# A mixed recurrence and expert kernel: the opening in another order, gating by two wide products, loads and early weight splits re-planned

## The chip, the cores and the metric

The kernel runs on one core of a Trainium2 chip. The metric is the device time in microseconds (us), taken as the median of several executions.

## What is computed

Two stages. The first is a gated recurrence (B = 2, H = 8, S = 768, D = 40), the second a dense mixture of four experts (1536 tokens, 320 to 1024 to 320 columns):

```python
m_new = max(f[t] + m, i[t]); f_stab = exp(f[t] + m - m_new); i_stab = exp(i[t] - m_new)
C = f_stab * C + i_stab * outer(v[t], k[t]);  n = f_stab * n + i_stab * k[t]
y[t] = sigmoid(o_gate[t]) * (C @ q[t]) / max(abs(n @ q[t]), 1.0)

x = y, heads side by side: (1536, 320);  p = domain_probs / (sum(domain_probs) + 1e-9)
out = sum over e of p[:, e] * (relu(x @ w1[e]) @ w2[e])
```

## The kernel before

**Units.** The tokens are cut into NT = 12 units of L = 128 (a chunk of one batch, all eight heads). Units 0 and 1 are the first chunks of the two batches and have no earlier state. For a unit k, `decays` (ScalarE) computes exponentials of gate sums into dec_w, one half being four heads; `causal` (GpSimd) masks them; `scores` (TensorE) multiplies queries and keys; `probs` (VectorE, DVE) multiplies scores and decays; `outputs` (TensorE) multiplies by the values, and from unit 2 on adds the part of the carried state; `additions` makes what the unit adds to the state from kw, which `weigh_keys` (GpSimd) prepares. `denominator` and `gate_x` (DVE) divide, and multiply by the sigmoid of the output gate, which `gate_open` (ScalarE) writes in place in y_acc. `transpose_x` turns the result; `xt_high` (ScalarE) and `xt_low` (DVE) split it into a high and a low part for products in reduced-precision fp32.

**Experts.** The weights of one expert are eight blocks of 128 hidden columns; a pair of blocks (704 KB) is one transfer into w_raw, which holds RAW_PAIRS = 3 pairs. `split_high` (ScalarE) rounds a block to w_hi, `split_low` (GpSimd) takes the rest in two pieces, 384 columns for the up product and 320 for the down product. Work is cut into SLOTS = 128 slots, sixteen groups of eight; the first three groups have two units each. In a slot M, `up(M+2)` (later M+1) makes the hidden values (eight matmuls, for two units of 256 columns), `relu` (ScalarE) and `hidden_low` (DVE) split them, and `down(M)` adds to acc_ps. After the eighth slot of a group `add_expert` (DVE) puts acc_ps into y_acc.

**Order.** Each engine runs a list written by hand, in order; semaphores tie the lists together. T0 says at which slot a unit starts (unit 2 at 3, unit 3 at 7, unit 4 at 16): its decays run at slots T0-1 and T0, the scores at T0 and T0+2, additions and outputs at T0+3, gate_x at T0+4, transposes at T0+6. EARLY_SPLITS says which weight blocks are split in slots 0 to 5. All loads but one are issued by SyncE (SP), so a wait in its list holds up every load behind it. Weight pair p waits until w_lo_done says that the pair three before it is split.

**The opening.** SyncE issues the gates, the scores' operands of units 0 and 1, keys and values, o_gate of units 0 to 3 (one transfer), and weight pair 0. `gate_steps` and `gate_sums` make the gate sums, first for units 0 and 1 (16 rows, gate tiles 0) and then for the ten others (80 rows, gate tiles 1), whose running maximum comes by five small transfers into m_u. TensorE runs `keep_clock` products, matmuls whose result is not used, between the steps. ScalarE holds one table of functions at a time; going from Exp to Sigmoid or back is an ACT_TABLE_LOAD. The second o_gate transfer (units 4 to 11, 1280 KB) lands on y_acc[:, 4:NT], where the gates of the opening lie until m_moved.

## Time and profile before

| | |
|---|---|
| median of 3 runs | 444.98 us (443.33 to 447.54) |
| the profiled execution | 445.01 us, span 443.3 us |
| TensorE (PE) busy | 97% of the span |
| VectorE (DVE), ScalarE (ACT), GpSimd (POOL) busy | 40%, 37%, 37% |
| read from and written to HBM | 44.79 MB, 2.05 MB |

Times in the trace count from the start of the span. PE is the matmul, PEld the weight load beside it; SPq is SyncE's queue. A number such as L908 is a line of the kernel: L908 is the up product, L925 down, L866 and L874 outputs, L847 additions, L820 scores, L886 to L888 the transposes, L789 keep_clock, L464 a decay, L613 probs, L644 gate_x, L384 and L386 the two pieces of split_low, L623 the split of queries and keys, L694 add_expert, L308 the second o_gate transfer. The granted clock is given as a share of the full clock.

### The profile page before, as it was taken

The page shows a single profiled execution, that of the slowest core. Times are in us where ns is not written, and L with a number is a line of the kernel's source. Part 1 is how long each engine was busy: PE and PEld are TensorE (multiplying, and loading weights), DVE is VectorE, ACT ScalarE, POOL GpSimd, SP SyncE. Part 2 cuts the span into 40 slices and gives each one's busy share as a digit, 9 for nine tenths or more (in the row PEclk, how much of TensorE's full clock was granted, in tenths as well). Part 3 has the DMA queues.
Part 4 walks back from the last instruction along what each step waited for, and adds up shares of the span by engine and source line. Part 5 has one row for each costly group of instructions (what it writes and reads, how often), then busy time and mean ns, then how long its engine had stood idle before and what let it go on. Part 6 is the DMA issues. An engine that isn't in the chain of part 4 may idle for free.

```text
span 443.3 us, 7101 instructions
## 1 busy us (share of the span) xinstructions
PE 429.0 (97%) x2716; PEld 412.8 (93%) x2716; DVE 175.9 (40%) x419; ACT 164.1 (37%) x332; POOL 164.3 (37%) x193
## 2 busy tenths in 40 slices
PE   8998689999999999999999999999999999999997
PEld 7887689999999999999999999999999999999996
DVE  6632144656564465653724323232313223122132
ACT  3656337557344382542412243124311233111111
POOL 4538763469453585521301066006500145100000
PEclk9899779999999999999999999999999999999999
DMA  8769688826985159740000024102220010001010
GB/s 234 236 182 267 248 241 241 203 65 172 288 187 151 67 149 257 189 138 6 0 1 1 0 74 136 53 0 92 106 67 0 1 65 1 0 1 59 1 59 31
DMA packets 25589, 47.33 MB, mean 107 GB/s; under 512 B 1971, under 2 KB 18788, under 8 KB 24468
## 3 DMA queue, kind: packets, MB, share of 16 engines
q1 hardware_dynamic: 25412, 46.86, 37.1%
q8 instruction: 22, 0.36, 0.3%
q14 instruction: 11, 0.09, 0.1%
q10 hardware_dynamic: 144, 0.02, 0.0%
HBM read 44.79 MB, written 2.05 MB: 106 GB/s over the span
## 4 chain that ended last, share of the span: by engine, by line
PE 87%; DMA 4%; DVE 3%; SPq 3%; ACT 1%; issue 1%; POOL 1%; DVEq 0%; ACTq 0%
PE hid_ps L908 38%; PE acc_ps L925 32%; PE out_ps L866 4%; PE score_ps L925 3%; PE add_ps L847 2%; DMA w_raw<-in_w_b 2%; PE out_ps L874 2%; PE score_ps L825 1%; PE hid_ps L789 1%; DMA raw<-in_qk_a 1%; PE score_ps L820 1%; DMA m_u<-y_acc 1%; SPq L308 1%; PE acc_ps L908 1%; DVE prob L613 1%
## 5 line engine op out<-in xcount | busy, mean ns | idle before, releaser
L678 DVE SCALAR_TENSOR_TENSOR h_lo<-hid_ps,h_hi 128x384 fp32r<-128x384 f32 (+2 forms) x120 | 68.0, 566 | 243.2 <-ACT h_hi L499 243.1
L499 ACT ACTIVATE h_hi<-hid_ps 128x384 fp32r<-128x384 f32 (+2 forms) x120 | 59.8, 498 | 246.5 <-PE hid_ps L908 246.0
L925 PE MATMUL acc_ps<-w_hi,h_hi 128*128 128x320 f32 x352 | 110.9, 315 | 1.3 <-DVE y_acc L694 1.2
L925 PE MATMUL acc_ps<-w_hi,h_lo 128*128 128x320 f32 x352 | 108.8, 309 | 0.0
L925 PE MATMUL acc_ps<-w_lo,h_hi 128*128 128x320 f32 x352 | 108.5, 308 | 0.0
L908 PE MATMUL hid_ps<-xt_hi,w_hi 128*128 128x384 f32 (+2 forms) x360 | 104.8, 345 | 2.4 <-issue 1.7
L384 POOL TENSOR_TENSOR w_lo<-w_raw,w_hi 128x384 fp32r<-128x384 f32 x56 | 61.1, 1091 | 117.6 <-ACT w_hi L485 117.6
L908 PE MATMUL hid_ps<-xt_hi,w_lo 128*128 128x384 f32 (+2 forms) x360 | 102.3, 341 | 0.0
L908 PEld LDWEIGHTS hid_ps<-xt_hi,w_lo 128*128 128x128 f32 x360 | 65.7, 190 | 4.0
L925 PEld LDWEIGHTS acc_ps<-w_hi,h_hi 128*128 128x128 f32 x352 | 66.5, 189 | 3.1 <-issue 1.4
L925 PEld LDWEIGHTS acc_ps<-w_lo,h_hi 128*128 128x128 f32 x352 | 66.4, 189 | 1.4
L908 PEld LDWEIGHTS hid_ps<-xt_hi,w_hi 128*128 128x128 f32 x360 | 62.6, 189 | 4.7 <-issue 2.4
L925 PEld LDWEIGHTS acc_ps<-w_hi,h_lo 128*128 128x128 f32 x352 | 66.2, 188 | 0.0
L908 PE MATMUL hid_ps<-xt_lo,w_hi 128*128 128x384 f32 (+2 forms) x240 | 63.0, 343 | 0.0
L386 POOL TENSOR_TENSOR w_lo<-w_raw,w_hi 128x320 fp32r<-128x320 f32 x56 | 50.0, 893 | 0.0
L485 ACT ACTIVATE w_hi<-w_raw 128x704 fp32r<-128x704 f32 x56 | 43.6, 782 | 6.4 <-DMA w_raw<-in_w_b 6.4
L908 PEld LDWEIGHTS hid_ps<-xt_lo,w_hi 128*128 128x128 f32 x240 | 43.0, 190 | 2.9
L364 POOL TENSOR_SCALAR_AFFINE_SELECT dec_w<-dec_w 128x512 f32<-128x512 f32 x24 | 15.3, 636 | 68.2 <-ACT dec_w L464 68.2
L866 PEld LDWEIGHTS out_ps<-kv,prob 128*128 128x128 f32 x176 | 22.7, 206 | 3.7 <-DVE prob L613 3.7
L866 PE MATMUL out_ps<-kv,prob 128*128 128x41 f32 x176 | 22.7, 306 | 3.4 <-DVE prob L613 3.4
L464 ACT ACTIVATE dec_w<-g_all,w_tok 128x128 f32<-128x128 f32 x80 | 25.4, 391 | 0.0
L623 DVE TENSOR_TENSOR split_qk<-raw,split_qk 40x1024 fp32r<-40x1024 f32 x16 | 22.4, 1398 | 0.2
(156 smaller groups left out, 384.2 us busy)
## 6 DMA issues: line engine op xcount, KB each, us to landing
w_raw<-in_w_b SPq DMA_DIRECT2D x28, 704.0 KB, 4.7
raw<-in_qk_s SPq DMA_DIRECT2D x8, 960.0 KB
g_all<-g_dram SPq DMA_DIRECT2D x10, 512.0 KB, 9.1
kv<-in_kv_n SPq DMA_DIRECT2D x12, 320.0 KB, 7.1
out_y<-y_acc SPq DMA_DIRECT2D x12, 160.0 KB, 1.9
q_pack<-in_q_p SPq DMA_DIRECT2D x10, 180.0 KB, 9.3
carry<-g_dram SPq DMA_DIRECT2D x30, 60.0 KB
y_acc<-in_o_n SPq DMA_DIRECT2D x1, 1280.0 KB, 12.0
```

Source lines behind the costliest of these rows:

```text
L364: nc.gpsimd.affine_select(out=d, in_=d, compare_op=ALU.is_ge, fill=0.0, base=0, pattern=[[0, HALF], [1, L]], channel_multiplier=-1).then_i ...
L384: nc.gpsimd.tensor_tensor(w_lo[:, f, 0:384], w_raw[:, at, 0:384], w_hi[:, f, 0:384].bitcast(fp32), ALU.subtract)
L386: nc.gpsimd.tensor_tensor(w_lo[:, f, 384:WB], w_raw[:, at, 384:WB], w_hi[:, f, 384:WB].bitcast(fp32), ALU.subtract).then_inc(w_lo_done, 1)
L464: last = nc.scalar.activation(dec_w[:, half, a, :], e, ACT.Exp, bias=w_tok[:, k * H + h:k * H + h + 1])
L485: nc.scalar.activation(w_hi[:, f, :], w_raw[:, at, :], ACT.Copy).then_inc(w_hi_done, 1)
L499: nc.scalar.activation(h_hi[:, M % RING, 0:cols], hid_bank(M)[:, 0:cols], ACT.Relu).then_inc(hid_hi, 1)
L623: nc.vector.tensor_tensor(hi, raw[rows, kept(k), t, :, :], hi.bitcast(fp32), ALU.subtract)\
L678: nc.vector.scalar_tensor_tensor(h_lo[:, M % RING, 0:cols], hid_bank(M)[:, 0:cols], 0.0, h_hi[:, M % RING, 0:cols].bitcast(fp32), ALU.max, ...
L847: last = nc.tensor.matmul(bank[0:KS, first * DA:(first + n) * DA], kw[:, kept(k), KS * g:KS * (g + 1)], values(k, first, n), start=True, s ...
L866: last = nc.tensor.matmul(bank[:, h * DA:(h + 1) * DA], prob[:, kept(k), h // HALF, h % HALF, :], values(k, h, 1).rearrange("p h e -> p (h ...
L908: last = nc.tensor.matmul(hid_bank(M)[:, 0:tiles * L], w, x, start=(i == 0), stop=(i == len(terms) - 1))
L925: last = nc.tensor.matmul(acc_ps[t][:, 0:DM], x, w, start=(f == 0 and i == 0), stop=(f == NF - 1 and i == 2))
```

## The change

- SyncE: o_gate of units 0 to 3 comes in two transfers right behind the gates. Weight pair 2 moves ahead of the scores' operands of unit 2; those of unit 3 and q of unit 3 move up behind them, and keys and values of unit 2, with their waits for out_done and add_done, ahead of pair 3. Keys and values of unit 3 stand ahead of g 2, and g 3 behind pair 4. The second o_gate transfer moves to slot 9, pairs 8, 9 and 10 to slots 12, 14 and 16, and a unit's loads from its slot T0+5 to T0+6.
- ScalarE: the sigmoids of units 0 to 3 come first, then the exponentials. Unit 1's decays go into g_all[:, 1], so they no longer wait for unit 0's products. Blocks 0 to 3 are split ahead of xt_high(0). The later sigmoids move from slots 9 and 10 to 13 and 14.
- DVE: all four products of the opening come ahead of gate_steps(1), the scan of gate_sums is a function of its own, and domain probabilities come last. `denominator` and `gate_x` are one function: one wide product with the sigmoid, one wide product with the reciprocals, instead of eight. For blocks 2 to 15 the down piece of the low part is made here (`split_down_low`), no longer on GpSimd.
- GpSimd: split_low(0) ahead of weigh_keys; blocks 2 to 15 only the up piece.
- TensorE: exponents first, scores(0,0) behind them; ten keep_clock products at the start and three later, where there were nine and twenty-two; key turn ahead of outputs(0); additions(0) and (1) behind the transposes, ahead of up(0). In `up` the low weights come ahead of the low part of x, and each is waited for where it is first used.

```diff
+DN_FIRST, DN_END = 2, 16
+LATER_PAIRS = {12: 8, 14: 9, 16: 10}
...
+        def dec(k, half):
+
+            return g_all[:, 1, half * HALF:(half + 1) * HALF, :] if k == 1 else dec_w[:, half, :, :]
...
             sp.dma_start(fi_sb, fi_rows).then_inc(gates_in, 16)
+            sp.dma_start(y_acc[:, 0:2, :], o_n[:, 0:2, :]).then_inc(o_in[0], 16)
+            sp.dma_start(y_acc[:, 2:4, :], o_n[:, 2:4, :]).then_inc(o_in[1], 16)
             load_scores(sp, 0)
             load_scores(sp, 1)
             load_kv(sp, 0)
-            sp.dma_start(y_acc[:, 0:4, :], o_n[:, 0:4, :]).then_inc(o_in[0], 16)
             load_kv(sp, 1)
 
             def load_pair(p):
 
                 wait_if(sp, w_lo_done, 2 * (p - RAW_PAIRS) + 2)
+                if halved_low(2 * (p - RAW_PAIRS)):
+                    sp.wait_ge(w_dn_done, 2 * (p - RAW_PAIRS) + 2 - DN_FIRST)
...
             load_pair(1)
+            load_pair(2)
             reload_scores(2)
             load_q(2)
-            load_pair(2)
+            reload_scores(3)
+            load_q(3)
+            sp.wait_ge(out_done, 1)
+            sp.wait_ge(add_done, 1)
+            load_kv(sp, 2)
             load_pair(3)
...
-            sp.wait_ge(out_done, 1)
-            sp.wait_ge(add_done, 1)
-            load_kv(sp, 2)
+            sp.wait_ge(out_done, 2)
+            sp.wait_ge(add_done, 2)
+            load_kv(sp, 3)
             sp.wait_ge(gate_tiles[1]["stored"], 2 * 16)
             load_g(2)
             load_carry(2)
             load_pair(4)
-            reload_scores(3)
-            sp.wait_ge(out_done, 2)
-            sp.wait_ge(add_done, 2)
-            load_kv(sp, 3)
             load_g(3)
-            load_q(3)
             load_carry(3)
-            sp.wait_ge(m_moved, 16 * (NC - 1))
-            sp.dma_start(y_acc[:, 4:NT, :], o_n[:, 4:NT, :]).then_inc(o_in[1], 16)
...
+                if M == T0[3] + 2:
+                    sp.wait_ge(m_moved, 16 * (NC - 1))
+                    sp.dma_start(y_acc[:, 4:NT, :], o_n[:, 4:NT, :]).then_inc(o_in[2], 16)
...
             causal(1, 1)
+            split_low(0)
             weigh_keys(0)
             weigh_keys(1)
-            for w in range(FIRST):
+            for w in range(1, FIRST):
                 split_low(w)
...
+            gate_open(0, 2)
+            gate_open(2, 2)
+            nc.scalar.activation(table_turn[:, 1:2], m_sb[:, 0:1], ACT.Exp)
             decays(0, 0)
...
             key_exp(0)
-            gate_open(0, 2)
             split_high(0, None)
             split_high(1, None)
+            split_high(2, None)
+            split_high(3, None)
             xt_high(0)
-            gate_open(2, 2)
             xt_high(1)
             relu(0)
-            split_high(2, None)
             relu(1)
-            split_high(3, None)
...
-            def denominator(k):
+            def gate_x(k):
+
 
                 dve.wait_ge(out_done, k + 1)
+                dve.wait_ge(sig_ready, k // 2 + 1 if k < 4 else k // 4 + 2)
+                wait_if(dve, xt_ps, k - 1)
                 total = out_bank.get(k, out_ps)[:, 0:H * DA].rearrange("p (h e) -> p h e", h=H)
+                x = x_nat[:, kept(k), :].rearrange("p (h d) -> p h d", h=H)
                 nc.vector.tensor_scalar(floor[:, :], total[:, :, D], 1.0, None, ALU.max).then_inc(floor_ready, 1)
+                nc.vector.tensor_tensor(x, total[:, :, 0:D], y_acc[:, k, :].rearrange("p (h d) -> p h d", h=H),
+                                        ALU.mult).then_inc(x_gated, 1)
...
+                nc.vector.tensor_tensor(x, x, rden[:, :].unsqueeze(2).broadcast_to([L, H, D]), ALU.mult)\
+                    .then_inc(x_ready, 1)
+
+            def split_down_low(w):
+
+                at, f = (w // 2) % RAW_PAIRS * 2 + w % 2, w % NF
+                dve.wait_ge(w_hi_done, w + 1)
+                nc.vector.tensor_tensor(w_lo[:, f, 384:WB], w_raw[:, at, 384:WB], w_hi[:, f, 384:WB].bitcast(fp32),
+                                        ALU.subtract).then_inc(w_dn_done, 1)
...
+            probs(0, 0)
+            probs(0, 1)
+            probs(1, 0)
+            probs(1, 1)
+            copy_keys(0, 0, U0, acc_ps[2])
+            dve.wait_ge(units_in, 16)
+            dve.wait_ge(m_moved, 16 * (NC - 1))
+            gate_steps(1, fi_u[:, 0, :], fi_u[:, 1, :], m_u[:, 0:L], m_u[:, 1:L + 1])
+            gate_x(0)
+            gate_scan(1)
+            gate_x(1)
+            xt_low(0)
+            xt_low(1)
+            gate_sums(1)
...
+                for w in blocks_to_split(M - 1) if M > 0 else []:
+                    if halved_low(w):
+                        split_down_low(w)
...
                 if first_of_load(M):
                     pe.wait_ge(w_hi_done, NF * load + f + 1)
-                    pe.wait_ge(w_lo_done, NF * load + f + 1)
                 if f == 0:
-                    pe.wait_ge(xt_done, first + tiles)
+                    pe.wait_ge(xt_hi_done, first + tiles)
...
                 for i, (w, x) in enumerate(terms):
+                    if i == 2 and first_of_load(M):
+                        pe.wait_ge(w_lo_done, NF * load + f + 1)
+                    if i == 4 and f == 0:
+                        pe.wait_ge(xt_done, first + tiles)
...
-            keep_clock(9)
-            scores(0, 0)
+            keep_clock(10)
             pe.wait_ge(ident_ready, 2)
             pe.wait_ge(g0["ready"], 1)
             turn(g0, "w", acc_ps[2], 0, U0, "w_ps")
             exponents_first(0, 0)
             exponents_first(0, 1)
-            scores(0, 1)
+            scores(0, 0)
             exponents_first(1, 0)
             exponents_first(1, 1)
+            scores(0, 1)
             scores(1, 0)
             scores(1, 1)
-            keep_clock(4)
-            outputs(0)
             pe.wait_ge(g0["exp"], 1)
             pe.wait_ge(g0["w_tok"], 1)
             turn(g0, "key", acc_ps[2], U0, U0, "key_ps")
-            keep_clock(4)
+            outputs(0)
             outputs(1)
             transpose_x(0)
-            keep_clock(8)
+            additions(0)
+            keep_clock(1)
             transpose_x(1)
-            keep_clock(6)
+            additions(1)
+            keep_clock(2)
             up(0)
...
             up(1)
-            additions(0)
-            additions(1)
```

## Rows read from the trace of the kernel before

**Rows 1.** The page: busy us (share of the span) xinstructions of each engine.
```profile
PE 429.0 (97%) x2716; PEld 412.8 (93%) x2716; DVE 175.9 (40%) x419; ACT 164.1 (37%) x332; POOL 164.3 (37%) x193
```

**Rows 2.** Stretches: us; busy PE, PEld, DVE, ACT, POOL (xinstructions); granted clock; DMA share; GB/s.
```profile
28.83:48.27 19.44, 17.27 (x117) 15.88 (x116) 4.27 (x12) 10.30 (x23) 14.41 (x17) 1.00 1.05 293
48.27:51.71 3.44, 0.00 (x2) 0.00 (x1) 1.08 (x3) 2.17 (x5) 1.31 (x2) 0.81 0.84 341
51.71:60.25 8.54, 8.54 (x36) 8.18 (x36) 0.75 (x3) 3.42 (x11) 5.65 (x8) 0.50 0.53 149
...
61.17:101.00 39.83, 37.04 (x281) 36.14 (x280) 22.92 (x64) 23.29 (x45) 21.30 (x24) 1.00 0.65 173
101.00:443.30 342.30, 339.37 (x2121) 327.46 (x2120) 127.95 (x275) 111.25 (x219) 107.28 (x117) 1.00 0.27 76
```

**Rows 3.** The chain that ended last, in order of time: start, us, piece; slots 8 to 14.
```profile
65.56 0.87 PE score_ps L820 x4
...
69.46 1.19 PE add_ps L847 x6
70.65 1.73 PE out_ps L866 x16
72.38 0.69 PE out_ps L874 x6
...
80.84 0.88 PE acc_ps L925 x6
81.73 0.96 PE acc_ps L908 x8
```

**Rows 4.** The timeline of the opening: start us, us, instructions; first a piece of the chain.
```profile
1.85 4.21 DMA raw<-in_qk_a
...
8.03 2.18 ACT L464 ACTIVATE dec_w<-acc_ps,w_tok 128x128 f32<-128x128 f32 x8 [5.29 <-PE acc_ps L797]
...
13.33 1.28 ACT L442 ACT_TABLE_LOAD   x1
...
15.44 1.28 DVE L613 TENSOR_TENSOR prob<-acc_ps,dec_w 128x512 f32<-128x512 f32 x2
...
16.94 1.97 PE L866 MATMUL acc_ps<-kv,prob 128*128 128x41 f32 x16 [1.09 <-DVE key_w L597]
...
17.34 1.43 DVE L644 SCALAR_TENSOR_TENSOR x_nat<-out_ps,rden,y_acc 128x40 f32<-128x40 f32 x8
...
22.18 0.42 PE L886 MATMUL acc_ps<-ident,x_nat 128*128 128x128 f32 x1
```

**Rows 5.** Busy time by single us around the first fall of the clock, columns as in rows 2.
```profile
19.00:20.00 1.00, 1.00 (x9) 1.00 (x9) 0.90 (x6) 0.59 (x2) 1.00 (x2) 0.84 0.92 323
...
23.00:24.00 1.00, 1.00 (x11) 1.00 (x10) 0.42 (x2) 0.49 (x1) 0.00 (x0) 0.95 0.87 220
```

**Rows 6.** The chain around weight pair 5, and transfers: KB each, median us to landing.
```profile
35.81 3.03 SPq L308
...
38.88 10.64 DMA w_raw<-in_w_b
...
g_all<-g_dram SPq DMA_DIRECT2D x10, 512.0 KB, 9.1
...
y_acc<-in_o_n SPq DMA_DIRECT2D x1, 1280.0 KB, 12.0
...
y_acc<-in_o_n SPq DMA_DIRECT2D x1, 640.0 KB, 6.6
```

**Rows 7.** One line's instructions (ns min/median/max), and the timeline of a collision.
```profile
L386 POOL TENSOR_TENSOR w_lo<-w_raw,w_hi x56: 850/872/1848, 19.3 to 377.5; 128x320 fp32r<-128x320 f32 x56
...
109.86 1.82 DVE L623 TENSOR_TENSOR split_qk<-raw,split_qk 40x1024 fp32r<-40x1024 f32 x1
...
110.54 2.00 POOL L384 TENSOR_TENSOR w_lo<-w_raw,w_hi 128x384 fp32r<-128x384 f32 x1
```

**Rows 8.** TensorE's waits, 24 to 110 us: who for whom, total us, times, longest.
```profile
PE acc_ps L925 <- DVE y_acc L694: 1.2, 1, 1.2
```

More of the change, by code:

```diff
@@ L181, in build @@
         gates_in, units_in, dp_in = sem("gates_in"), sem("units_in"), sem("dp_in")
-        o_in = [sem(f"o_in{i}") for i in range(2)]
+        o_in = [sem(f"o_in{i}") for i in range(3)]
         w_in = [sem(f"w_in{i}") for i in range(RAW_PAIRS)]
@@ L362, in causal @@
                 pool.sem_inc(mask_turn, 1)
-                d = dec_w[:, half, :, :]
+                d = dec(k, half)
                 nc.gpsimd.affine_select(out=d, in_=d, compare_op=ALU.is_ge, fill=0.0, base=0,
@@ L463, in decays @@
                     e = bank[:, a * L:(a + 1) * L] if k < B else g_all[:, kept(k), h, :]
-                    last = nc.scalar.activation(dec_w[:, half, a, :], e, ACT.Exp, bias=w_tok[:, k * H + h:k * H + h + 1])
+                    last = nc.scalar.activation(dec(k, half)[:, a, :], e, ACT.Exp, bias=w_tok[:, k * H + h:k * H + h + 1])
                 last.then_inc(d_exp, 1)
@@ L574, in gate_sums @@
                     .then_inc(step, 1)
+            def gate_sums(n):
+                gt = gate_tiles[n]
+                g, j, gg, step = gt["g"], gt["j"], gt["gg"], gt["step"]
                 dve.wait_ge(step, 5)
@@ L602, in _ @@
             gate_steps(0, fi_sb[:, 0, 0:L], fi_sb[:, 1, 0:L], m_sb[:, 0:L], m_sb[:, 1:L + 1])
+            gate_scan(0)
             gate_sums(0)
@@ L699, in add_expert @@
                                                        ALU.mult, ALU.add).then_inc(acc_free, 1)
+            probs(0, 0)
[12 more added lines that the diff above has]
+            gate_sums(1)
+            hidden_low(0)
+            copy_tokens(1, U0, U1, out_ps)
+            hidden_low(1)
+            keep_heads(0)
+            keep_heads(1)
+            for w in range(DN_FIRST, FIRST):
+                split_down_low(w)
             dve.wait_ge(dp_in, 16)
```

78 lines of the change are left out of this document (32 added, 46 removed).

## The prediction

> **What bounds the kernel now.** I read the busy times first: TensorE is busy for 429.0 of 443.3 us [rows 1], so only time in which it stands still or runs slowly can be won. The busy time by stretches shows where that is. From 101 us to the end it is busy for 339.37 of 342.30 us, all at full clock, and nothing in the diff shortens a matmul there. From 28.83 to 48.27 it is busy for 17.27 of 19.44; from 48.27 to 51.71 it does nothing; from 51.71 to 60.25 it is busy, but at a granted clock of 0.50, which is the lower of its two levels (1.2 GHz) [rows 2]. I call pass M of the main loop slot M. Slot 0 begins with up(2) at 28.83, slot 8 with up(10) at 61.17.
>
> What do slots 0 to 7 cost without a loss? The chain of work gives 0.96 for up, 0.88 for down, 0.87 for half the scores, and 1.19 + 1.73 + 0.69 = 3.6 for a unit's additions and outputs [rows 3]. Eight ups and downs are 14.7, three halves of scores 2.6, one unit's additions and outputs 3.6, the key turn and the diagonal product of slot 1 about 0.4 (an estimate, two or three small matmuls of the 0.23 to 0.5 kind [rows 3, 4]): 21.3 us. They took 61.17 - 28.83 = 32.3. So **11.0 us are lost**: 2.2 in small gaps before 48.27, 3.4 in the gap, 4.3 as half of the 8.54 slow us, and some 1.1 in gaps and half-clock edges around them. The last part is the difference, not read.
>
> Who causes the gap? The chain names it. SyncE was busy for 3.03 us issuing the second o_gate transfer (1280 KB) at 35.81, issued weight pair 5 behind it at 38.88, and that landed 10.64 us later, at 49.5 [rows 6]. ScalarE takes that pair in slot 4; the relus and the decays of unit 2 stand behind it in its queue, then the DVE product, then outputs(2) on TensorE. The idle time let the clock fall.
>
> **The opening, step by step.** Before: the decays run from 8.03 (eight in 2.18, so 1.1 a half), wait once for a product to free dec_w, and end with key_exp at 13.3, where the table of the sigmoid is loaded (1.28) [rows 4]. After: the two small o_gate transfers go right behind the gates, 320 KB each. The 640 KB of before took 6.6 us behind 1.2 MB of other loads; fi, 96 KB and first in the queue, and the scores' operands (416 KB) bound the other side, the latter with 4.21 us from issue to landing [rows 4, 6]. I take landings at 5.5 and 6.5. A decay of 128 columns takes 0.27, so a sigmoid of 640 takes at most five times that, 1.4, and with one fixed part instead of five about half, 0.7 (an estimate). The sigmoids end at 7.2, the exp table at 8.5, the small activation at 8.7. Decays: 8.7 to 13.1, with no wait between, since unit 1 now writes g_all. key_exp ends at 13.5. So this part is level with before: the removed wait pays for the early sigmoid. With 6.6 us per landing it would start 2.3 later.
>
> The Trainium skill, ScalarE: Activation LUTs, section Table sets: the hidden batching unit, puts a switch at about 2.7 us. This trace disagrees, with 1.28 [rows 4]; by the page the decays would begin 1.4 later and the sum below would be 1.4 higher.
>
> From there, TensorE: key turn at 13.6, outputs(0) 13.8 to 15.7 and outputs(1) right behind, to 17.6, each like the 1.97 of before; before, outputs(1) started at 16.94, because the DVE stood in front of unit 1's products waiting for m_u and did gate_steps(1) first; its two products ran at 15.44 to 16.72 [rows 4]. That is 1.3 earlier. gate_x: eight products of 1.43 together become two wide ones. A 128x512 product is half of 1.28, 0.64 to 0.69, so 320 columns are 0.45 to 0.5 each; one lies in the shadow of the floor and denominator chain, so x is ready 0.6 earlier per unit [rows 4]. x(0) is ready at 17.1, inside outputs(1), turned by 18.1. x(1): done at 17.6, gate_scan(1) in front, ready at 19.1; additions(0) fill TensorE until 19.4; turned by 20.0, where before its turn began at 22.18 after eight keep_clock products. additions(1) to 21.2, two keep_clock products, up(0) and up(1) from 21.7 to 23.7, the turn of w: slot 0 at 24.0, 4.8 before the 28.83 of now [rows 3, 4]. That includes the 2.4 us of additions that now stand after up(1).
>
> **The clock.** It fell to 0.84 in 19 to 20 and was back at 0.95 in 23 to 24, after outputs(1) and an idle us ahead of them, and in spite of the keep_clock products [rows 4, 5]. After the change there are 13 such products instead of 31, and ten of them stand at the start; from 13.6 to 21 TensorE has only narrow outputs, transposes and additions. I expect the fall. A slow stretch of 3.2 us as in 20 to 23 costs half, 1.6; one of 8.54, as later, 4.3 [rows 2, 5]. Before, the slow stretch covered mostly filler; now it covers work. I take 2.0, and slot 0 at 26.0.
>
> **Slots 0 to 7.** The second o_gate transfer goes to slot 9, behind pairs 5, 6 and 7 and scores 4. scores 3 and q 3 move ahead of pair 3. In the queue of SyncE pair 3 now stands behind waits for out_done 1 and add_done 1 (about 19.4, which is as late as its own wait for w_lo 2, 19.9), and pair 5 behind pair 4 (27.4: w_lo 4, and the down halves of blocks 2 and 3, which the DVE does only after keep_heads, about 26.6), g 3 and three carries. It is issued at about 31.4 instead of 38.88 and has no 1280 KB ahead. At the 12.0 us that 1280 KB took in a full queue, 704 KB take 6.6 [rows 6], so it lands at 38 or, in an emptier one, at 36; slot 4 on ScalarE comes at 36. g 2 is issued at 25.5 to 26 (its store waits for ready 2 of unit gates 1, about 22.8, and now for out_done 2), and with the 9.1 us of such a transfer [rows 6] it lands by 35; without queueing, by 31. decays(2,0) stand in ScalarE's queue at slot 2, before the splits 6 and 7. That can hold up(6) by up to 2. I take 1.5 us of new stalls in all, range 0 to 4.
>
> The down halves (14 blocks): GpSimd loses 14 pieces of 0.87 [rows 7]. The DVE pays: a 320-column piece is between 0.40 (320/512 of a product's 0.64 [rows 4]) and 0.57 (320/1024 of the 1.82 of a split [rows 7]), I take 0.5; it is on no path but in slot 7, where it delays add_expert by 0.5 while the shorter gate_x gives back 0.6. There TensorE waited 1.2 us for y_acc; I keep that [rows 8]. One thing speaks against this edit: a DVE split over 1024 columns ran from 109.86 to 111.68, and the 384-column GpSimd split that began within it took 2.00, where the 0.87 of 320 columns would give 1.05 [rows 7]. So the two engines do not fully overlap, and GpSimd gets back 0.87 - 0.5, or 0.4 a block. The cover that hides it is GpSimd's idle time (164 of 443 busy [rows 1]); gone, it would cost 14 x 0.5 = 7 us at worst. The Trainium skill, SBUF — State Buffer, section Who interferes with whom, says that a DVE instruction with two SBUF inputs and a GpSimd one that reads SBUF exclude each other; by that rule, the trace agrees, and the sum stays as it is.
>
> Slot 8 is then at 26.0 + 21.3 + 1.5 = 48.8 instead of 61.17: **12.4 us earlier**.
>
> **Behind slot 8.** From 61.17 to 101 TensorE stands still for 2.8 us [rows 2]. The o_gate transfer issued in slot 9 (by 50) must land by slot 13, at 48.8 + 5 x 1.84 + 0.87 + 0.3 + 3.6 = 62.8; unit 4's loads and scores 5 follow it. 1280 KB took 12.0 us in the profile of before with a full queue; that is just enough. ScalarE then does two table loads and two sigmoids in slots 13 and 14, 5.3 us in one run, with a relu between; TensorE is two slots (3.7 us) ahead of its needs, so up to 1 us can show. up waits for xt_lo only at its fifth product, which gives 0.4 back in slot 14. Net 0. LATER_PAIRS move pairs 8 to 10 to slots 12 to 16; blocks 16 and up are split from slot 18, so it costs nothing; the cover is some 7 us of slots.
>
> **The sum.** 2.8 in the opening + 11.0 - 1.5 in slots 0 to 7 = 12.3, taken as 12.4 with the unrounded slots. The profiled execution took 445.01 us for a span of 443.3, which is the median of the runs, 444.98. 445.0 - 12.4 = **432.6**. Its own range is 430 to 436.
>
> **The rivals.**
> - No fall of the clock and no new stall: 445.0 - 12.4 - 2.0 - 1.5 = 429.1; with some of the later 2.8 us saved too, 427.5. For it: dense outputs and additions at 69.46 to 73.07 did not lower the clock. Against: no such rest with so little wide work. Chance 0.2.
> - The clock stays low for long in the opening (4.3 instead of 2.0), and o_gate lands late (2.3) or pair 5 and g 2 stall for 4 instead of 1.5: 432.6 + 2.3 + 2.4 = 437.3 (2.3 from the clock, 2.4 from one of the other two). For it: every landing above is a guess under a full queue. Chance 0.2.
> - The stall only moves: o_gate lands after slot 13, and relu(16) stands behind it. Price: the gap and the slow clock again, 3.4 + 4.3 = 7.7, so 440.3, no difference by a measurement. It ends slower than before only if TensorE's wait there is 4.7 us longer than the 3.4, that is if o_gate lands after about 73 instead of 62.8. Chance 0.1, of which 0.02 slower.
> - The change does not do what it says, as the DVE and SyncE serve slots 0 to 7 no sooner: only the opening's 2.8 remain, 442.2. Against: the 1280 KB do leave that place. Chance 0.03.
>
> The forecast has 0.47. A measurement of this kernel can tell about 1%, 4.4 us, from no change. Faster by over 1% (under 440.5): the first three and a part of the fourth, 0.91; within 1%: 0.07; slower: 0.02. The range is 428 to 439: it leaves out the lower end of the first rival and the last two.
>
> **What would show it.** In the profile after: the first decays near 8.7, slot 0 near 26 and slot 8 near 49; no gap over 2 us between; weight pair 5 landed before 38; x_nat products of 0.5; the clock low for 2 to 5 us around 20; GpSimd's busy time lower by 12 us and DVE's higher by 0 to 5. I am wrong if the decays start after 10, if a wait of ScalarE for g_all or o_gate tops the waits, or if TensorE is idle for over 3 us behind slot 8.

## The result, and the profile after

The changed kernel takes 441.72 us (median of 7 runs, 439.58 to 442.37) where the kernel before took 445.21 (7 runs). The ratio is 0.9892, 95% interval 0.9849 to 0.9935: about 1.1% faster. The forecast of 432.6 is missed, and the time lies outside its range of 428 to 439. The profiled execution took 440.28 us for a span of 438.6.

The page of after, then its stretches. Slot 0 begins at 27.47 and slot 8 at 52.79; columns as in [rows 2].

```profile
PE 423.7 (97%) x2680; PEld 408.6 (93%) x2680; DVE 184.5 (42%) x361; ACT 163.2 (37%) x332; POOL 155.9 (36%) x179
```

```profile
27.47:52.79 25.32, 23.11 (x157) 22.42 (x156) 16.31 (x35) 14.81 (x38) 14.03 (x14) 0.93 0.68 210
52.79:101.00 48.21, 43.44 (x311) 42.49 (x309) 27.98 (x58) 28.71 (x57) 25.03 (x27) 0.96 0.70 196
...
101.00:438.60 337.60, 334.66 (x2092) 322.75 (x2091) 122.18 (x226) 106.58 (x210) 103.12 (x112) 1.00 0.27 75
```

Against [rows 2] the gap at 48.27 and the 8.54 slow us behind it are gone, and slot 8 comes 8.4 us earlier. But from 52.79 to 101 TensorE is idle for 48.21 - 43.44 = 4.8 us, where it was 2.8 before in the stretch that also starts at slot 8, and the granted clock is 0.96, not 1.00. The waits of TensorE name the places (who waits for whom: total us, times, longest). The 1.2 of [rows 8] has become 2.6, and the other three are new:

```profile
PE hid_ps L927 <- DVE x_nat L677: 2.6, 1, 2.6
PE acc_ps L971 <- DVE y_acc L732: 2.6, 1, 2.6
PE out_ps L1020 <- DVE decay_diag L793: 2.2, 1, 2.2
PE acc_ps L971 <- DVE y_acc L736: 1.2, 1, 1.2
```

All are waits for the DVE: from the top, in the opening, at slot 8, in slot 1 and at slot 16. In after's lines L927 is the first transpose, L971 the down product, L1020 the product with the decays' diagonal, L668 and L677 the two wide products of gate_x, L684 the down piece on the DVE, L732 and L736 add_expert. TensorE itself waits for a transfer only once before slot 8, for 0.2 us; one transfer still paces it by way of the DVE, as shown below. Pair 5 in ScalarE's timeline and the o_gate transfers (KB, median us to landing) answer [rows 6]:

```profile
43.23 0.79 ACT L511 ACTIVATE w_hi<-w_raw 128x704 fp32r<-128x704 f32 x1 [0.25 <-DMA w_raw<-in_w_b]
```

```profile
y_acc<-in_o_n SPq DMA_DIRECT2D x1, 1280.0 KB, 11.3
y_acc<-in_o_n SPq DMA_DIRECT2D x2, 320.0 KB, 3.5
```

**The opening of after**, start and us, of DVE and GpSimd (POOL):

```profile
14.49 1.00 POOL L405 TENSOR_TENSOR w_lo<-w_raw,w_hi 128x384 fp32r<-128x384 f32 x1 [1.93 <-ACT w_hi L511]
...
14.89 0.75 DVE L588 TENSOR_TENSOR fm<-fi_u,m_u 80x128 f32<-80x128 f32 x1 [1.45 <-DMA m_u<-y_acc]
15.45 0.91 POOL L410 TENSOR_TENSOR w_lo<-w_raw,w_hi 128x320 fp32r<-128x320 f32 x1
15.56 0.95 DVE L589 TENSOR_TENSOR j<-fi_u,m_u 80x128 f32<-80x128 f32 x1
...
17.24 0.47 DVE L668 TENSOR_TENSOR x_nat<-out_ps,y_acc 128x320 f32<-128x320 f32 x1
...
17.79 0.99 POOL L405 TENSOR_TENSOR w_lo<-w_raw,w_hi 128x384 fp32r<-128x384 f32 x1
...
18.13 1.00 DVE L677 TENSOR_TENSOR x_nat<-x_nat,rden 128x320 f32<-128x320 f32 x1
...
19.05 1.07 DVE L600 TENSOR_TENSOR_SCAN gg<-ones,g 80x127 f32<-80x127 f32 x1
```

The first wide product, with one input in PSUM, takes 0.47. The second, same size, with both in SBUF and GpSimd reading beside it, takes 1.00, and 0.93 in the median of all twelve units (min/median/max):

```profile
L677 DVE TENSOR_TENSOR x_nat<-x_nat,rden x12: 492/934/1229, 18.1 to 228.4; 128x320 f32<-128x320 f32 x12
```

TensorE was done with both outputs at 16.5 and waited until 19.18. Its stretches of two us (columns as in [rows 2]) show what followed: the low clock from 16 to 26, the first and the last of five here, and 6.9 us of work in them.

```profile
16.00:18.00 2.00, 0.54 (x3) 0.39 (x2) 1.97 (x6) 1.28 (x2) 2.00 (x4) 0.50 1.04 272
...
24.00:26.00 2.00, 2.00 (x12) 2.00 (x11) 0.94 (x4) 0.00 (x0) 0.00 (x0) 0.53 0.81 317
```

The chain of work that ended last shows one thing more that stands ahead of the products:

```profile
10.49 4.31 DMA m_u<-y_acc
```

outputs(0) were done at 14.4, but the DVE does gate_steps(1) before gate_x(0); they wait for this transfer until 14.89 and then, beside GpSimd, run until 17.24. Before, the transfer landed at about the same time (14.7). No run puts gate_steps(1) behind gate_x(0), so what this order costs is not measured.

**Slot 8 of after.** From the DVE's product to the wait that ends on add_expert:

```profile
53.70 1.23 DVE L677 TENSOR_TENSOR x_nat<-x_nat,rden 128x320 f32<-128x320 f32 x1
...
54.54 0.97 POOL L396 TENSOR_TENSOR kw<-kv,key_w 128x320 f32<-128x320 f32 x1
...
54.85 1.01 DVE L684 TENSOR_TENSOR w_lo<-w_raw,w_hi 128x320 fp32r<-128x320 f32 x1
...
55.78 1.00 DVE L732 TENSOR_SCALAR y_acc<-acc_ps,pn 128x320 f32<-128x320 f32 x2
...
56.46 0.49 PE L971 MATMUL acc_ps<-w_hi,h_hi 128*128 128x320 f32 x1 [2.55 <-DVE y_acc L732]
```

**Slot 1 of after.** The DVE does the down pieces and the domain probabilities while the diagonal is what TensorE needs:

```profile
29.24 0.88 DVE L684 TENSOR_TENSOR w_lo<-w_raw,w_hi 128x320 fp32r<-128x320 f32 x2
...
30.27 0.91 DVE L763 TENSOR_SCALAR dp_inv<-dp_sum 128x12 f32<-128x12 f32 x1
...
32.06 0.60 DVE L793 TENSOR_SCALAR decay_diag<-ident,decay_u 80x80 f32<-80x80 f32 x1
...
32.71 0.69 PE L1020 MATMUL out_ps<-decay_diag,ones 80*120 80x80 f32 x2 [2.21 <-DVE decay_diag L793]
```

### The profile page after: what moved, and what is told of

Same layout as the page of the kernel before. It is cut to its first block, busy times and chain, and to the rows that moved or that the text cites. A ratio compares the mean times of both kernels' runs of the same rounds, so it can differ in the third digit from the quotient of the medians.

```text
span 438.6 us, 6982 instructions
## 1 busy us (share of the span) xinstructions
PE 423.7 (97%) x2680; PEld 408.6 (93%) x2680; DVE 184.5 (42%) x361; ACT 163.2 (37%) x332; POOL 155.9 (36%) x179
## 4 chain that ended last, share of the span: by engine, by line
PE 90%; DVE 5%; issue 2%; DMA 2%; ACT 1%; SPq 1%; DVEq 0%; ACTq 0%
PE hid_ps L952 39%; PE acc_ps L971 35%; PE out_ps L907 4%; PE score_ps L971 3%; PE add_ps L888 3%; PE out_ps L915 2%; PE score_ps L866 1%; PE acc_ps L952 1%; DMA m_u<-y_acc 1%; PE score_ps L861 1%; DVE x_nat L677 1%; DMA y_acc<-in_fi_rows 1%; SPq L300 1%; ACT h_hi L525 0%; DVE w_lo L684 0%
## 5 line engine op out<-in xcount | busy, mean ns | idle before, releaser
L971 PE MATMUL acc_ps<-w_hi,h_hi 128*128 128x320 f32 x352 | 111.3, 316 | 3.8 <-DVE y_acc L732 2.6
L971 PE MATMUL acc_ps<-w_hi,h_lo 128*128 128x320 f32 x352 | 109.4, 311 | 0.0
L971 PE MATMUL acc_ps<-w_lo,h_hi 128*128 128x320 f32 x352 | 109.0, 310 | 0.0
L952 PE MATMUL hid_ps<-xt_hi,w_lo 128*128 128x384 f32 (+2 forms) x360 | 103.9, 343 | 0.0
L971 PEld LDWEIGHTS acc_ps<-w_hi,h_hi 128*128 128x128 f32 x352 | 66.6, 189 | 5.7 <-issue 2.7
L971 PEld LDWEIGHTS acc_ps<-w_lo,h_hi 128*128 128x128 f32 x352 | 66.7, 190 | 1.3
L971 PEld LDWEIGHTS acc_ps<-w_hi,h_lo 128*128 128x128 f32 x352 | 66.6, 189 | 0.0
L410 POOL TENSOR_TENSOR w_lo<-w_raw,w_hi 128x320 fp32r<-128x320 f32 x42 | 38.0, 905 | 0.0
L907 PEld LDWEIGHTS out_ps<-kv,prob 128*128 128x128 f32 x176 | 21.1, 194 | 0.0
L907 PE MATMUL out_ps<-kv,prob 128*128 128x41 f32 x176 | 21.1, 296 | 0.0
## 6 DMA issues: line engine op xcount, KB each, us to landing
y_acc<-in_o_n SPq DMA_DIRECT2D x1, 1280.0 KB, 11.3
```

The costliest lines, as they stand in the source:

```text
L410: nc.gpsimd.tensor_tensor(w_lo[:, f, 384:WB], w_raw[:, at, 384:WB], w_hi[:, f, 384:WB].bitcast(fp32), ALU.subtract).then_inc(w_lo_done, 1)
L907: last = nc.tensor.matmul(bank[:, h * DA:(h + 1) * DA], prob[:, kept(k), h // HALF, h % HALF, :], values(k, h, 1).rearrange("p h e -> p (h ...
L952: last = nc.tensor.matmul(hid_bank(M)[:, 0:tiles * L], w, x, start=(i == 0), stop=(i == len(terms) - 1))
L971: last = nc.tensor.matmul(acc_ps[t][:, 0:DM], x, w, start=(f == 0 and i == 0), stop=(f == NF - 1 and i == 2))
```

## The experiments

My theory after the result (A): the loss is the DVE's. Its instructions with two inputs in SBUF are held up while GpSimd reads, and its list puts work that nobody waits for ahead of work that TensorE waits for. The rivals: the loads (B), and the clock, which falls in the opening whatever the DVE does (C). The start of relu(M), the first ScalarE instruction on the result of up(M), serves as a ruler: relu(0) ends the opening, relu(10) stands in slot 8, and from relu(24) to the end each of these kernels takes 339.9 to 340.0 us. Each row is one profiled execution.

| | relu(0) | relu(10) | relu(24) |
|---|---|---|---|
| before | 25.69 | 62.32 | 103.30 |
| after | 26.61 | 53.95 | 98.61 |
| after once more (same kernel) | 29.97 | 55.77 | 100.46 |
| before with the load order alone | 25.25 | 54.05 | 98.45 |
| after, second product from PSUM | 26.92 | 54.12 | 95.67 |
| after, fillers in the opening | 25.80 | 53.01 | 96.15 |
| after, DVE order | 27.25 | 50.64 | 92.83 |
| DVE order and PSUM | 24.64 | 48.02 | 88.83 |
| DVE order, PSUM, sigmoids in slot 10 | 27.77 | 51.37 | 90.76 |
| the same with four more fillers | 24.86 | 48.54 | 87.91 |

**The second product reads PSUM.** No DVE product of gate_x has two SBUF inputs now.

```diff
-                nc.vector.tensor_tensor(x, total[:, :, 0:D], y_acc[:, k, :].rearrange("p (h d) -> p h d", h=H),
+                gated = total[:, :, 0:D]
+                nc.vector.tensor_tensor(gated, gated, y_acc[:, k, :].rearrange("p (h d) -> p h d", h=H),
...
-                nc.vector.tensor_tensor(x, x, rden[:, :].unsqueeze(2).broadcast_to([L, H, D]), ALU.mult)\
+                nc.vector.tensor_tensor(x, gated, rden[:, :].unsqueeze(2).broadcast_to([L, H, D]), ALU.mult)\
```

> The changed kernel, but the first wide product of gate_x is written back into its PSUM bank, so that the second one reads PSUM and the reciprocals instead of two SBUF tiles. Same operations, same columns. Theory A (the wide product collides with GpSimd's reads of SBUF): the second product falls from 1.00 and 1.23 us for units 0 and 1, and 1.23 for unit 2, to about 0.5 each; x(0) is ready 0.5 earlier, x(1) 1.2 earlier, the wait of 2.6 us at slot 8 shrinks to about 1.9, and the span falls from 438.6 to about 437. Theory B (the DVE simply has too much to do in the wrong order): durations and span stay within 0.3.

Measured: 436.9 us, ratio 0.9794 (0.9744 to 0.9844). The second product takes 0.49 in all twelve units with GpSimd as busy as before, the wait in slot 8 falls from 2.6 to 1.6, and no slow clock follows it (1.00 from 56 to 60, 0.57 in after). The gain lies behind slot 8: relu(0) and relu(10) are no earlier than in after, because in this execution most of the opening's early matmuls took double. The timeline of this kernel:

```profile
53.87 0.49 DVE L678 TENSOR_TENSOR x_nat<-out_ps,rden 128x320 f32<-128x320 f32 x1
```

**GpSimd doesn't read for blocks 0 to 3.**

```diff
+                if w < FIRST:
+                    nc.gpsimd.memset(w_lo[:, f, 0:384 if halved_low(w) else WB].bitcast(fp32), 0.0).then_inc(w_lo_done, 1)
+                    return
```

> The changed kernel, but for blocks 0 to 3 GpSimd fills the low part of the weights with zeros instead of subtracting, so it writes and reads nothing (these blocks' low part is left out of the result, and GpSimd's pieces are shorter). Theory A (collisions with GpSimd's reads): the three steps of gate_steps(1), 0.75, 0.95 and 0.81 us in the changed kernel, fall to 0.28 each as before the change, the wide products to 0.5; x(1) is turned near 20 instead of 22.3 and slot 0 begins near 25.5 instead of 27.5. Theory B (order, or the lower clock alone): the DVE's durations stay as they are.

Measured: 441.32 us, one run. The durations are as A has them: 0.28, 0.28 and 0.81 for the gate steps (the last ran beside weigh_keys), 0.49 for both second products, 0.41 for the scan. Together 2.8 us, where after has 0.75 + 0.95 + 0.81 + 1.00 + 1.07 + 1.23 = 5.8. But the clock was 0.50 from 10 to 26 and ate the gain: relu(0) came at 29.10, not earlier as expected. So the low clock (C) costs by itself, and here it was low before TensorE first waited for gate_x.

**Down pieces back on GpSimd.**

```diff
-DN_FIRST, DN_END = 2, 16
+DN_FIRST, DN_END = 4, 4
```

> The changed kernel, but the down halves of blocks 2 to 15 go back to GpSimd. Theory A (a DVE piece with two SBUF inputs blocks and is blocked): the DVE's wait-free stretch at slot 8 shortens by 1.0 and the wait there falls from 2.6 to about 1.5, slot 1's wait from 2.2 to about 1.3; but GpSimd's w_lo come 0.9 a block later, which costs nothing as they are early in slots 0 to 7. Span about 436.5. Theory C (the pieces were a relief that slots 0 to 7 need): span 439 to 442, new waits of up() for w_lo.

Measured: 442.95 us, ratio 0.9964 (0.9926 to 1.0003), no different from before. The expected gain at slot 8 (a wait of 1.5, span 436.5) did not come, and the reason is the strongest evidence for A. Its timeline in slot 8, of the DVE's product, GpSimd's masking that was under way when it began, all of GpSimd that follows, add_expert, and TensorE behind it:

```profile
51.24 0.65 POOL L385 TENSOR_SCALAR_AFFINE_SELECT dec_w<-dec_w 128x512 f32<-128x512 f32 x1
51.51 5.91 DVE L677 TENSOR_TENSOR x_nat<-x_nat,rden 128x320 f32<-128x320 f32 x1
...
51.85 1.01 POOL L405 TENSOR_TENSOR w_lo<-w_raw,w_hi 128x384 fp32r<-128x384 f32 x1
...
52.80 0.87 POOL L410 TENSOR_TENSOR w_lo<-w_raw,w_hi 128x320 fp32r<-128x320 f32 x1
53.62 0.73 POOL L396 TENSOR_TENSOR kw<-kv,key_w 128x320 f32<-128x320 f32 x1
...
54.30 1.00 POOL L405 TENSOR_TENSOR w_lo<-w_raw,w_hi 128x384 fp32r<-128x384 f32 x1
55.26 0.87 POOL L410 TENSOR_TENSOR w_lo<-w_raw,w_hi 128x320 fp32r<-128x320 f32 x1
56.07 1.00 POOL L418 TENSOR_TENSOR q_pack<-q_pack,carry 120x384 f32<-120x384 f32 x1
...
57.34 1.00 DVE L732 TENSOR_SCALAR y_acc<-acc_ps,pn 128x320 f32<-128x320 f32 x2
...
58.03 0.61 PE L971 MATMUL acc_ps<-w_hi,h_hi 128*128 128x320 f32 x1 [6.31 <-DVE y_acc L732]
```

One product of 0.5 us takes 5.91: it ends at 57.42, when GpSimd's run of six more reading instructions has ended (57.07). TensorE waits 6.3 us there.

**The same with the PSUM product.** The edit of the first experiment and this one together.

> The changed kernel with gate_x through PSUM and the down pieces of blocks 2 to 15 back on GpSimd. Theory A (the wide product with two SBUF inputs is held up until GpSimd's run of reads ends; it took 5.91 us with the down pieces on GpSimd): without such a product the second product stays at 0.5 us however busy GpSimd is, the wait of 6.3 us at slot 8 falls below 1, and the span is at or below the 435.6 of gate_x through PSUM alone. Theory C (GpSimd itself is the bound with the down pieces back): the wait at slot 8 stays over 4 us, or moves to w_lo, span 439 or more.

Measured: 435.16 us, ratio 0.977 (0.9709 to 0.983); the wait in slot 8 is 0.9, from 6.3. With the PSUM product the time is the same whether the down pieces are on the DVE (0.9794) or on GpSimd (0.977). So the move of the down pieces pays, as far as these runs show, only by breaking up GpSimd's runs.

**Order on the DVE.** Domain probabilities first of all, the down pieces of blocks 2 and 3 behind the diagonal, add_expert ahead of a slot's down piece.

```diff
+            dve.wait_ge(dp_in, 16)
+            nc.vector.tensor_reduce(dp_sum[:, :], dp[:, :, :], AX.X, ALU.add).then_inc(p_step, 1)
...
             probs(0, 0)
...
             keep_heads(1)
-            for w in range(DN_FIRST, FIRST):
-                split_down_low(w)
-            dve.wait_ge(dp_in, 16)
-            nc.vector.tensor_reduce(dp_sum[:, :], dp[:, :, :], AX.X, ALU.add).then_inc(p_step, 1)
...
-                for w in blocks_to_split(M - 1) if M > 0 else []:
-                    if halved_low(w):
-                        split_down_low(w)
                 if M % NF == NF - 1:
                     add_expert(M // NF)
+                for w in blocks_to_split(M - 1) if M > 0 else range(DN_FIRST, FIRST):
+                    if halved_low(w):
+                        split_down_low(w)
```

> The changed kernel with three moves in the DVE's list only: the domain probabilities back ahead of the first products, the down pieces of blocks 2 and 3 behind the diagonal of slot 0, and add_expert ahead of the down piece in the last slot of a group. Theory B (order): TensorE's wait of 2.2 us for the diagonal in slot 1 and the slow clock behind it go (3 to 3.5 us by slot 4), and the wait of 2.6 at slot 8 falls to 1.6; span 438.6 - 4.5 = about 434. Theory A alone (collisions, wherever they stand): the pieces collide elsewhere, span within 1.5 of 438.6.

Measured: 434.11 us, ratio 0.977 (0.9734 to 0.9805). The wait in slot 1 is gone, the one in slot 8 is 1.6, and the clock no longer falls in the slots. relu(24) comes 5.8 us earlier than in after, and 6.4 counted from relu(0), for 3.2 us of waits removed (2.2 and 1.0). The rest fits the slow clock that used to follow them: 0.59 from 32 to 36 and 0.57 from 56 to 60 are 4 x 0.41 + 4 x 0.43 = 3.4 (an estimate). In the opening TensorE still waits 2.9 us for x(0). The three moves were made together, so their shares are not measured.

**Filler products in the opening.**

```diff
             outputs(0)
+            keep_clock(4)
             outputs(1)
+            keep_clock(10)
             transpose_x(0)
             additions(0)
-            keep_clock(1)
+            keep_clock(4)
```

> The changed kernel with keep_clock products back in the opening: four between outputs(0) and outputs(1), ten behind outputs(1), four instead of one behind additions(0). Theory C (the lower clock in the opening costs): the granted clock stays 1.00 until 26 or is low only for part of it, slot 0 begins near 25.5 instead of 27.5, span about 437. If the DVE sets the opening (theory A): the clock may stay high, but x(1) comes no earlier, and only the transposes, additions and first up gain, 1.3 us at most.

Measured: 441.52 us, ratio 0.9868 (0.9804 to 0.9932). The clock stayed at 1.00 to 30, but relu(0) came only 0.8 earlier, because the DVE still sets the opening: x(1) is no earlier. The first transpose of x(1) in this kernel and in after:

```profile
22.62 0.33 PE L927 MATMUL acc_ps<-ident,x_nat 128*128 128x128 f32 x1 [0.32 <-DVE x_nat L677]
```

```profile
22.27 0.47 PE L927 MATMUL acc_ps<-ident,x_nat 128*128 128x128 f32 x1 [0.48 <-DVE x_nat L677]
```

From here to relu(0) this kernel takes 3.2 us, after 4.3. So the low clock of after's opening cost the path about 1.2 us; what else makes slot 0 late is x(1).

**Sigmoids at the end of slot 10**, both behind one table load (after has slots 13 and 14).

```diff
-                if M in (T0[4] - 3, T0[4] - 2):
-                    gate_open(4 + 4 * (M - T0[4] + 3), 4)
-                if M == T0[4] - 2:
+                if M == T0[3] + 3:
+                    gate_open(4, 4)
+                    gate_open(8, 4)
```

> The changed kernel, but the later sigmoids with both table loads stand at the end of slot 10 on ScalarE (where it was idle for 4 us, from 64 to 68) instead of slots 13 and 14. If they cost the time behind slot 13, as relu(17) stands behind them: TensorE's wait of 1.2 us for add_expert's y_acc at slot 16 goes, span 1.2 to 2 lower, about 437. If o_gate (issued at 47.4, 11.3 us to landing) is not there by then, ScalarE waits at slot 10 instead and the span is equal or higher.

Measured: 439.81 us, ratio 0.9893 (0.9846 to 0.994), no different from after. But from relu(10) to relu(24) it takes 43.2, where after takes 44.7, and the 1.2 wait of slot 16 is gone; the opening of this profile was 1.7 later.

**Before, with the load order alone.** The second o_gate transfer to slot 9, the later sigmoids to slots 13 and 14, nothing else.

```diff
-            sp.wait_ge(m_moved, 16 * (NC - 1))
-            sp.dma_start(y_acc[:, 4:NT, :], o_n[:, 4:NT, :]).then_inc(o_in[1], 16)
...
+                if M == T0[3] + 2:
+                    sp.wait_ge(m_moved, 16 * (NC - 1))
+                    sp.dma_start(y_acc[:, 4:NT, :], o_n[:, 4:NT, :]).then_inc(o_in[1], 16)
```

> The kernel before the change, with one part of the change alone: the second o_gate transfer in slot 9 and the later sigmoids in slots 13 and 14. If this transfer made the gap at 48.27 to 51.71 (the prediction's step): weight pair 5 lands 3 us or more before 49.5, the gap and the slow clock behind it go, span 443.3 - 7.7 + 1.2 (sigmoids in slots 13 and 14) = about 437, so nearly the whole gain of the change by this edit alone. If the pair's own wait for w_lo and a full queue made it: pair 5 is issued before 37 but lands after 46, span 441 or more.

Measured: 443.19 us, ratio 0.994 (0.9894 to 0.9985), and so not the expected gain in time; the profiled execution took 440.15, the second fastest of ten. In it the gap is gone: pair 5 is issued at 36.25 instead of 38.88 and landed by 44.8 instead of 49.5. relu(10) comes at 54.05, in after at 53.95. So this move alone gives the whole gain at slot 8; everything else in the change adds up to 0.1 us there, as it makes relu(0) 1.4 later and the way from relu(0) to relu(10) 1.5 shorter (one profile of each). ScalarE still waits for pair 5, for 2.1 us and not into the path. Its timeline:

```profile
44.83 0.79 ACT L486 ACTIVATE w_hi<-w_raw 128x704 fp32r<-128x704 f32 x1 [2.11 <-DMA w_raw<-in_w_b]
```

Behind slot 8 this kernel too loses 3.4 us against before, with waits of 1.6 (slot 16) and 1.5 (slot 8) for add_expert and a granted clock of 0.62 from 80 to 84:

```profile
PE acc_ps L926 <- DVE y_acc L699: 1.6, 1, 1.6
```

This kernel has none of the change's edits on the DVE. So the moved transfer and the late sigmoids lost nearly as much behind slot 8 by themselves as the whole change did.

**Combinations.** First PSUM, order, sigmoids and fillers; then without the fillers; then without the sigmoids too. The last in this group is the changed kernel once more.

> The changed kernel with four edits together: gate_x through PSUM, the DVE's order, the keep_clock products and the sigmoids in slot 10. If their gains add (2.9 of the first as measured, 3 to 4.5 of the order, 1 of the clock, 1.2 of the sigmoids): span 430 to 432. If one stall hides behind another, more than 433.

> The changed kernel with gate_x through PSUM, the DVE's order and the sigmoids in slot 10, without the keep_clock products. From the order's span of 432.8: minus 1.5 at slot 8 (the product no longer waits there), minus 1.4 for the sigmoids (as relu 10 to relu 24 gained 1.4 in that run), span 429 to 431; where the matmuls of the opening run at half speed, 1.7 to 2.5 more.

> The changed kernel with gate_x through PSUM and the DVE's order, the sigmoids left in slots 13 and 14. If the sigmoids cost what relu 10 to relu 24 showed, 1.4 more than with them in slot 10: span 430.5 to 432.5. If not, the two kernels' spans agree within 0.5 where their openings agree.

> The changed kernel as it is, beside the others on one chip: median 440 to 442, span 438 to 441, and a wait of 2.2 us in slot 1 and 2.6 at slot 8 as in its first profile, whether or not the opening's matmuls run at half speed in this execution (relu(0) at 26.6, or 1.7 to 2.5 later).

Measured: 432.99 (ratio 0.9716, 0.9654 to 0.9778), **431.03 (0.9679, 0.9619 to 0.9739)**, 435.47 (0.9754, 0.9673 to 0.9835) and 440.52 (0.9872, 0.9793 to 0.9952). The fillers of the first show no gain. The intervals of the next two overlap; the profiles show what the sigmoids in slot 10 give, 39.4 instead of 40.8 from relu(10) to relu(24). The profiled execution without them, 430.52, was the fastest of its four. The repeat confirms the result of after and its three waits (2.2, 2.5, 1.2), with relu(0) at 29.97 instead of 26.61.

**Who slows the opening?** In the profiles with the new opening relu(0) lies between 24.6 and 30.0 (in one execution of the first combination at 36.4), because TensorE's matmuls there take double in some of them. The first suspect was TensorE's wait for the scores' operands raw 0, which land behind 640 KB of o_gate. Raw 0 first, in the best kernel and in the changed one; then the old load order with four fillers.

```diff
             sp.dma_start(fi_sb, fi_rows).then_inc(gates_in, 16)
+            load_scores(sp, 0)
             sp.dma_start(y_acc[:, 0:2, :], o_n[:, 0:2, :]).then_inc(o_in[0], 16)
             sp.dma_start(y_acc[:, 2:4, :], o_n[:, 2:4, :]).then_inc(o_in[1], 16)
-            load_scores(sp, 0)
```

```diff
             exponents_first(0, 1)
+            keep_clock(4)
             scores(0, 0)
```

> The fastest kernel so far (second product reads PSUM, opening's DVE order, later sigmoids in slot 10), with unit 0's raw scores (operands raw 0, 416 KB) issued ahead of the two small o_gate transfers (640 KB) instead of behind them. Theory A (TensorE's wait for raw 0 of 0.2 to 1.7 us is what lets the opening's matmuls fall to twice their time in some profiles): raw 0 lands at about 6 instead of 7.7 to 9.2, the exponents and scores take 1.1 us for four (not 2.07), relu(0) starts at or before 26; the decays start some 1 to 1.8 us later than 8, at 9.4, so of the gain over the fastest so far 0 to 2 us remains: 429 to 431. Rival B (the wait has nothing to do with it; the matmuls run at half speed in some executions whatever stands ahead): relu(0) is at 27 to 30 in this profile or the next one, and the time is the fastest one's plus the 1 us by which the decays are later, 432. Against the kernel before: A 0.965, B 0.971.

> The changed kernel with the same one move: raw 0 issued ahead of the two small o_gate transfers. Theory A: raw 0 lands at about 6, full-speed matmuls in the opening, relu(0) at 26 to 27 (the changed kernel's profile had 26.6 with raw at 7.7, its second profile 30.0 with the half-speed opening), time 438 to 440. Rival B: relu(0) 27.5 to 31, time 441 to 443, since the decays are later by 1 to 1.8 us.

> The fastest kernel so far with four keep_clock products (about 0.95 us at full speed) ahead of the first scores, so that TensorE's wait for raw 0 is partly filled and the load order stays. Theory A: the matmuls behind it take 1.1 us for four, relu(0) at 25 to 26, time 429.5 to 430.5. Rival B: half speed comes anyway, the fillers cost 0.9 to 1.9 us more and relu(0) is at 28 to 30, time 431.5 to 433.

Measured: 432.74 (0.9733, 0.9679 to 0.9788), 441.8 (0.9934, 0.9902 to 0.9967) and **429.91 (0.968, 0.9626 to 0.9735)**. Four scores in the best kernel so far, in the one with raw 0 first and in the one with fillers, from their timelines:

```profile
9.19 2.07 PE L859 MATMUL score_ps<-raw 104*128 104x256 f32 x4 [1.67 <-DMA raw<-in_qk_a]
```

```profile
7.36 1.08 PE L859 MATMUL score_ps<-raw 104*128 104x256 f32 x4
...
11.82 2.61 PE L859 MATMUL acc_ps<-raw 104*128 104x256 f32 x8 [1.63 <-ACT dec_w L490]
...
15.32 3.64 PE L905 MATMUL out_ps<-kv,prob 128*128 128x41 f32 x16
```

```profile
8.24 1.08 PE L859 MATMUL score_ps<-raw 104*128 104x256 f32 x4
```

Raw 0 first removes the first wait and its doubling, as expected, and makes a new one: o_gate is later, so are the sigmoids and the decays, TensorE waits 1.6 for dec_w, and the outputs take 3.64 instead of 2.0. Neither kernel gains. With fillers ahead of the scores these matmuls ran at full speed (the granted clock fell only at 16) and relu(0) came at 24.86. That is one profile, and the ratio is the same as without them (0.968 and 0.9679), so I don't claim a gain from them. The wait is not the only cause either: the first experiment's opening was slow with no wait over 0.3 us after the start. And the same wait can be followed by either speed. The scores of after, and those of the kernel with the down pieces on GpSimd:

```profile
7.70 1.13 PE L861 MATMUL score_ps<-raw 104*128 104x256 f32 x4 [0.23 <-DMA raw<-in_qk_a]
```

```profile
7.71 1.72 PE L861 MATMUL score_ps<-raw 104*128 104x256 f32 x4 [0.23 <-DMA raw<-in_qk_a]
```

Up to here the two kernels do the same. Behind it the granted clock was 1.00 from 10 to 14 in the first and 0.50 in the second. What decides it stays open.

## Why the prediction was wrong, step by step

In the profiled execution the forecast is missed by 440.28 - 432.6 = 7.7 us. It falls on slot 0 (27.47 instead of 26.0: 1.5), on slots 0 to 7 (25.3 instead of 22.8: 2.5) and on what lies behind slot 8 (3.7 instead of 0).

- **The cause of the gap: right.** The kernel before with the load order alone shows it. Pair 5 was not issued at 31.4 but at 38.76, and came 0.25 us late for ScalarE; that it would land "at 38 or ... at 36" was wrong, and it didn't matter. The third rival's late o_gate did not come: issued at 47.38, it took 11.3 us, so it was there by 59.
- **The bare cost of slots 0 to 7, 21.3 us: right.** Measured are 25.3. Of these, 2.2 are the wait of slot 1, and a mean granted clock of 0.93 costs (1 - 0.93) x 25.3 = 1.8. That leaves 21.3. The failed term is "1.5 us of new stalls in all", where the wait and the clock behind it took 4.0: I looked for stalls in transfers, and they were in the DVE's list. That the down pieces are "on no path but in slot 7" was wrong. Blocks 2 and 3, with the domain probabilities that the change puts last, stand ahead of the diagonal of slot 1. I had not asked what is queued behind them.
- **The collision of DVE and GpSimd: the row was read, and in one direction only.** I took from [rows 7] that a DVE split stretches a GpSimd one, and priced GpSimd's loss. The other direction decides: the DVE's second wide product, the gate steps, the scan and the down piece wait for GpSimd. In the opening that is 5.8 - 2.8 = 3.0 us of DVE time, and x(1) is ready at 22.2 where I had 19.1 and turned by 23.2 where I had 20.0. In slot 8 the product takes 1.23, not the 0.45 to 0.5 of my sum, so "the shorter gate_x gives back 0.6" turned into a loss, and the 1.2 of [rows 8] that I kept became 2.6; the PSUM product alone and the DVE's order alone each leave 1.6, both together 0.9. The experiments with PSUM, without reads, and with down pieces on GpSimd show it from three sides. The Trainium skill, SBUF — State Buffer, section Who interferes with whom, has the rule and says that issue order decides who blocks; I cited it and wrote "the sum stays as it is". The trace of after agrees (1.23 where one input in PSUM gives 0.48), and these runs go beyond the page, which speaks of one instruction that waits until the other one is finished: the 5.91 us span six in a row behind the masking.
- **The clock: right that it falls, wrong in price and place.** I took 2.0 for the opening. In after 6.9 us of work lie in the slow stretch; half of that would be 3.4, but most of it lay in the shadow of the late DVE. By the run with fillers the path paid about 1.2. So the clock cost less than I took: slot 0 is late because x(1) was turned 3.2 later, of which 1.7 came back behind it. What the forecast lacked is that a new wait in the slots brings the low clock with it. In slots 1 and 8 waits of 2.2 and 2.6 were followed by means of 0.59 and 0.57 over 4 us; from relu(0) to relu(24) 6.4 us went with 3.2 us of waits.
- **The start of the decays: right and better.** They start at 7.62 instead of 8.7, as the small o_gate transfers landed in 3.5 us. outputs(1) end at 16.5, 1.1 us earlier than forecast, and TensorE then waited for the DVE.
- **Behind slot 8, "net 0": wrong.** The idle time grew by 2.0 us (from 2.8 to 4.8, over the 3 that I had named as a sign of being wrong), and the clock of 0.96 costs (1 - 0.96) x 48.2 = 1.9, together 3.9 for 3.7 measured. The wait of slot 8 is one part. The other is the place of the sigmoids in slots 13 and 14, where two table loads and the sigmoids hold ScalarE from 73.14 to 78.4; relu(17) and add_expert are late, and TensorE waits 1.2 us. I had said that "up to 1 us can show" and entered 0. In slot 10 they make TensorE wait nowhere. The kernel before with only the later transfer and the later sigmoids lost 3.4 here.
- **The rivals.** None was the one that came. The second (437.3) put a price of 4.3 on the opening's clock, where the path paid about 1.2, and its stalls into transfers. The fourth (442.2) has nearly the right time for a wrong reason: slots 0 to 7 were served sooner, and it was the opening that gave little. GpSimd's busy time fell by 8.4, not 12: the 14 down pieces gave their 12.0 (50.0 to 38.0), but other instructions of its list grew (the masks from 15.3 to 16.3, kw from 10.6 to 11.2); the rest of the difference is not traced.

With the DVE's order and the PSUM product slot 8 comes earlier than my 48.8 in the two profiles whose opening was fast: relu(10) is at 48.02 (sigmoids left in slots 13 and 14) and 48.54 (sigmoids in slot 10, four fillers) and follows the start of slot 8 by 1.2, so that is at 46.9 and 47.4. The median times with the sigmoids in slot 10 are 431.03 and 429.91, without that move 435.47. So a gain of the forecast size was there, but not in the change as made: it gave it back on the DVE and, by the place of the sigmoids, on ScalarE. How the two share it is known only roughly.

## What to carry over

When a wait is removed, list what each engine will do in the stretch that becomes free, in its own order, and ask of each entry who waits behind it; the loss here was three entries in the wrong place. Price an elementwise instruction by where its inputs lie: with two in SBUF and GpSimd reading, it took 0.93 in the median and up to 5.91 us here, and with the intermediate written back to PSUM 0.49 each time. The waits of TensorE of 2.2 and 2.6 us cost about twice that here, through the clock. It isn't a matter of length alone: behind a wait of 1.6 at slot 8 the clock stayed at 1.00 in two kernels, and behind one of 1.6 at slot 16 it fell in another (0.62 from 80 to 84).
